# Bucketed attention and two MLPs: queries and keys turned on the host, bits as plain float32 products on quarters of the array, values on halves of it in one long run for each three query tiles

## What is computed

```python
q_bits = (np.einsum('bhsd,dk->bhsk', q, proj) > 0).astype(np.int64)
k_bits = (np.einsum('bhsd,dk->bhsk', k, proj) > 0).astype(np.int64)
mask = q_bucket[:, :, :, None] == k_bucket[:, :, None, :]
scores = scale * np.matmul(q, k.transpose(0, 1, 3, 2))
scores = np.where(mask, scores, -1000000000.0)
scores = scores - np.max(scores, axis=-1, keepdims=True)
attn = np.exp(scores)
attn = attn / (np.sum(attn, axis=-1, keepdims=True) + 1e-09)
return np.matmul(attn, v).astype(np.float32)
```

## Time and profile before

| | us |
|---|---|
| median of 3 runs (817.24 to 818.34) | 817.36 |
| profiled execution, its own time | 818.54 |
| its span, first to last instruction | 816.8 |
| PE busy | 787.6 (96%) |
| DVE busy | 548.8 (67%) |
| ACT busy | 501.4 (61%) |
| POOL busy | 283.8 (35%) |

### The profile page before, as it was taken

One profiled execution on the slowest core, in us unless ns is written; L12 is line 12 of the kernel. 1 busy time (PEld: TensorE's weight loads), 2 busy tenths in 40 slices (PEclk: granted clock), 3 DMA queues, 4 the chain that ended last, 5 costly groups with the idle time before them and its releaser, 6 DMA issues.

```text
span 816.8 us, 13110 instructions
## 1 busy us (share of the span) xinstructions
PE 787.6 (96%) x3968; PEld 665.4 (81%) x3968; DVE 548.8 (67%) x929; ACT 501.4 (61%) x950; POOL 283.8 (35%) x457
## 2 busy tenths in 40 slices
PE   4999999999999889999999999999999999999998
PEld 4898888988888668888888888888888888888886
DVE  3899899989998678888988898893222322232223
ACT  2788887888889789877676688984222122212221
POOL 2887777877777844410000024442000000000000
PEclk9999999999999999999999999999999999999999
DMA  5221221222111233310000013331000100010001
GB/s 153 61 63 52 79 60 50 61 79 60 50 42 48 72 84 103 94 37 0 0 0 0 1 48 97 98 95 51 1 1 0 52 0 0 0 45 7 0 1 52
DMA packets 33568, 36.67 MB, mean 45 GB/s; under 512 B 3136, under 2 KB 25664, under 8 KB 33536
## 3 DMA queue, kind: packets, MB, share of 16 engines
q1 hardware_dynamic: 33536, 36.26, 15.7%
HBM read 26.22 MB, written 3.15 MB: 36 GB/s over the span
## 4 chain that ended last, share of the span: by engine, by line
PE 75%; DVE 8%; issue 7%; ACT 6%; POOL 2%; DMA 1%; ACTq 0%; DVEq 0%; SPq 0%; POOLq 0%
PE y_ps L954 32%; PE h_ps L888 10%; PE h_ps L889 10%; PE h_ps L887 10%; PE o_ps L866 4%; PE t_ps L854 3%; PE s_ps L844 2%; ACT probs L450 2%; ACT pt_hi L459 2%; DVE pt_lo L655 2%; PE s_ps L845 2%; DVE neg_max L641 2%; PE p_ps L817 1%; DVE q_main L635 1%; DVE o_pair L664 1%
## 5 line engine op out<-in xcount | busy, mean ns | idle before, releaser
L728 DVE SCALAR_TENSOR_TENSOR t_abs<-t_abs,h_ps 128x512 f32<-128x512 f32 x48 | 33.0, 688 | 187.1 <-ACT t_abs L525 187.1
L399 POOL TENSOR_TENSOR slot<-w_raw,slot 128x512 fp32r<-128x512 f32 x64 | 81.5, 1293 | 206.2 <-ACT slot L478 206.2
L525 ACT ACTIVATE t_abs<-h_ps,three_col 128x512 f32<-128x512 f32 x48 | 33.1, 689 | 191.1 <-PE h_ps L889 191.0
L887 PE MATMUL h_ps<-x_hi,slot 128*128 (+1 forms) x384 | 150.1, 391 | 0.2 <-DVE t_num L709 0.2
L889 PE MATMUL h_ps<-x_hi,slot 128*128 (+1 forms) x384 | 150.2, 391 | 0.0
L888 PE MATMUL h_ps<-x_lo,slot 128*128 (+1 forms) x384 | 150.0, 391 | 0.0
L954 PE MATMUL y_ps<-g_hi,slot 128*128 128x512 f32 x384 | 126.2, 390 | 0.4 <-DVE g_lo L734 0.4
L954 PE MATMUL y_ps<-slot,g_hi 128*128 128x512 f32 x384 | 118.3, 389 | 0.0
L450 ACT ACTIVATE probs<-s_ps,exp_bias,exp_scale 128x768 f32<-128x768 f32 x96 | 95.5, 995 | 35.4 <-POOL exp_bias L386 34.7
L655 DVE TENSOR_TENSOR pt_lo<-t_ps,pt_hi 128x384 fp32r<-128x384 f32 x192 | 97.3, 548 | 17.9 <-ACT pt_hi L459 16.8
L641 DVE TENSOR_REDUCE neg_max<-s_ps 128x1 f32<-128x768 f32 x96 | 91.5, 953 | 11.3 <-PE s_ps L845 10.0
(11 more groups left out here) (102 smaller groups left out, 1416.6 us busy)
## 6 DMA issues: line engine op xcount, KB each, us to landing
w_raw<-in_moe_w_in SPq DMA_DIRECT2D x32, 256.0 KB, 2.7
w_raw<-in_moe_w_out SPq DMA_DIRECT2D x32, 256.0 KB, 2.7
raw_qk<-in_q SPq DMA_DIRECT2D x16, 192.0 KB, 2.4
raw_qk<-in_k SPq DMA_DIRECT2D x16, 192.0 KB, 2.5
raw_v<-in_v SPq DMA_DIRECT2D x16, 192.0 KB, 2.4
q_main<-q_cross SPq DMA_DIRECT2D x16, 192.0 KB
k_main<-k_cross SPq DMA_DIRECT2D x16, 192.0 KB
out<-t_den SPq DMA_DIRECT2D x6, 256.0 KB, 2.1
```

What stands on the lines that cost most here:

```text
L399: nc.gpsimd.tensor_tensor(slots[f][:, j, 1, :], w_raw[j][:, :], slots[f][:, j, 0, :].bitcast(F32), ALU.subtract).then_inc(w_lo_made, 1)
L887: mm(h_ps[b][:, :], w_hi, x_hi[:, kt, cols], start=(kt == 0), stop=False)
```

## The change

The host hands over queries and keys as (batch, head, 64, 768), with the tokens in the order in which the kernel takes them. One head's queries (rows 0 to 63) and keys (rows 64 to 127) are one tile `raw`. ACT copies it as the high part into `q_main` (`split_hi`), POOL subtracts for the low part into `q_cross` (`split_lo`), and SP moves the halves to where the score products want them (`place_head`, four transfers, and `place_bits`, four). `project` takes `raw` and the unsplit `proj` as plain float32: four products a pair of 32 columns of weights each, on four different quarters of the array's columns. DVE makes all bits of a pair in one operation (`threshold`), which goes through a tile `bits`.

The probabilities are copied as plain float32, one half of each tile by ACT, the other by DVE (`take_turned`). `weigh` multiplies them with the unsplit values, 64 columns of weights for each head, head 0 on the left half of the array's columns, head 1 on the right half. The output is then already the two heads' rows of `x`, and ACT and DVE split it straight from PSUM, one group of three query tiles at a time (`upper_x`, `lower_x`). The work of pair i is done during pair i+1: twelve products behind each other at tiles 2 and 8, right behind the transposes of the step. The scale of the scores moves from the copy of the keys into `bias`, whose second operation now needs the result of the first. All pairs are written out, there is no loop in this stage. Five weight slots are split during pairs 2 to 6, the others during the first MLP steps.

```diff
-    def heads_view(x):
-        return x.rearrange("b h (p t) d -> (b h) p (t d)", p=P)
-
-    q_dram, k_dram, v_dram = heads_view(q), heads_view(k), heads_view(v)
+    q_dram, k_dram = (x.rearrange("b h d n -> (b h) d n") for x in (q, k))
+    v_dram = v.rearrange("b h (p t) d -> (b h) p (t d)", p=P)
...
+    WEIGH_AT = {2: (0, 1, 2, 3, 4, 5)}
+    PROJECT_AT = TILES + 2
+
+    LAST_WEIGH = {2: (0, (0, 1, 2, 3, 4, 5)), 8: (1, (0, 1, 2, 3, 4, 5))}
+    LAST_X = {6: 2 * PAIRS - 4, 11: 2 * PAIRS - 3}
+
+    EARLY_SLOTS = 5
+    EARLY_PAIR = PAIRS - 1 - EARLY_SLOTS
+    EARLY_AT = (4, 8)
...
+            def place_head(h):
+
+                u = h % 2
+                sp.wait_ge(hi_made, h + 1)
+                move(k_main[u][0:D, :], q_main[u][D:P, :]).then_inc(moved_in[u], 16)
+                move(k_cross[u][0:D, :], q_main[u][D:P, :]).then_inc(moved_in[u], 16)
+                if h > 0:
+                    sp.wait_ge(lo_made, h + 1)
+                    move(k_cross[u][D:P, :], q_cross[u][D:P, :]).then_inc(moved_in[u], 16)
+                    sp.wait_ge(moved_in[u], 48 * (h // 2 + 1) - (16 if u == 0 else 0))
+                move(q_cross[u][D:P, :], q_main[u][0:D, :]).then_inc(main_in[u], 16)
...
+            def place_bits(h):
+
+                i, u = divmod(h, 2)
+                sp.wait_ge(bits_made, i + 2 if h else 1)
+                for half in range(2):
+                    cols = slice(HALF * half, HALF * (half + 1))
+                    at = QUAD * (2 * u + half)
+                    move(q_main[u][D:KROWS, cols], bits[at:at + MASKROWS, :]).then_inc(main_in[u], 16)
+                    move(k_main[u][D:KROWS, cols], bits[at + MASKROWS:at + 2 * MASKROWS, :]).then_inc(main_in[u], 16)
...
-                nc.gpsimd.tensor_scalar(exp_scale[:, r:r + 1], neg, MATCHED, 1.0, ALU.is_lt, ALU.mult)
-                nc.gpsimd.tensor_scalar(exp_bias[:, r:r + 1], neg, MATCHED, neg, ALU.is_lt, ALU.mult)\
+                nc.gpsimd.tensor_scalar(exp_scale[:, r:r + 1], neg, MATCHED, SCALE, ALU.is_lt, ALU.mult)\
+                    .then_inc(matched, 1)
+                alone(matched, n + 1)
+                nc.gpsimd.tensor_scalar(exp_bias[:, r:r + 1], neg, exp_scale[:, r:r + 1], 1.0, ALU.mult, ALU.mult)\
                     .then_inc(biased, 1)
...
+                    if j % TILES == 1 and h + 1 < NHEAD:
+                        split_lo(h + 1)
...
+            def split_hi(h):
+
+                i, u = divmod(h, 2)
+                act.wait_ge(raw_in[i % 2][u], 32 * (i // 2 + 1))
+                after(act, scored, TILES * (h - 1))
+                nc.scalar.activation(q_main[u][:, :], raw[i % 2][u][:, :], ACT.Copy).then_inc(hi_made, 1)
...
+                if t == 0 and 3 <= h < NHEAD - 1:
+                    upper_x(h - 3)
+                if n >= 1:
+                    exponentials(n - 1, j - 1)
+                if t == 0 and h + 1 < NHEAD:
+                    split_hi(h + 1)
+                if n >= TURN_LAG:
+                    take_turned(n - TURN_LAG)
...
+            def take_turned(n):
+
+                i, j = divmod(n, 2 * TILES)
+                u, t = divmod(j, TILES)
+                dve.wait_ge(turned, 2 * n + 2)
+                freed_by(dve, i, u, t // GROUP)
+                c = P * (t % GROUP)
+                nc.vector.tensor_copy(pt(i, u, t // GROUP)[:, GROUP:TILES, c:c + P],
+                                      t_ps[1][:, 0:HALF].rearrange("p (k q) -> p k q", k=GROUP))\
+                    .then_inc(pt_dve_made, 1)
...
+                for half in range(2):
+                    at = QUAD * (2 * u + half)
+                    last = mm(p_ps[at:at + QUAD, 0:HALF], proj_pair[:, :],
+                              raw[i % 2][u][:, HALF * half:HALF * (half + 1)], start=True, stop=True)
...
+                for kt in some:
+                    for u in range(2):
+                        last = mm(weigh_bank(e)[D * u:D * (u + 1), 0:HALF], v_nat[i % 2][u][:, kt, :],
+                                  pt(i, u, g)[:, kt, :], start=(kt == 0), stop=(kt == TILES - 1))
...
+                scores(h, i, u, n, j, t)
+                if n >= TURN_LAG:
+                    for half in range(2):
+                        turn_probs(n - TURN_LAG, half)
+                if i == PAIRS - 1 and j in LAST_WEIGH:
+                    weigh(i - 1, *LAST_WEIGH[j])
+                if 1 <= i < PAIRS - 1 and t in WEIGH_AT:
+                    weigh(i - 1, u, WEIGH_AT[t])
+                if j == PROJECT_AT and i + 1 < PAIRS:
+                    project(i + 1, 0)
+                    project(i + 1, 1)
...
+            pe.wait_ge(x_ready, 2 * PAIRS - 2)
+            hidden(0, 0, 0, 0)
+            for n in (NTILE - 3, NTILE - 2):
+                for half in range(2):
+                    turn_probs(n, half)
+            weigh(PAIRS - 1, 0, tuple(range(TILES)))
+            for half in range(2):
+                turn_probs(NTILE - 1, half)
+            hidden(1, 0, 0, 1)
+            weigh(PAIRS - 1, 1, tuple(range(TILES)))
```

More of the change, by code:

```diff
@@ L374, in _, with split_lo @@
-            pool.wait_ge(first_split, 4)
-            pool.sem_inc(qk_step, 4)
-            for part in range(4):
-                split_qk(1, 0, 1, part)
+            def split_lo(h):
+                u = h % 2
+                alone(hi_made, h + 1)
+                nc.gpsimd.tensor_tensor(q_cross[u][:, :], raw[h // 2 % 2][u][:, :], q_main[u][:, :].bitcast(F32),
+                                        ALU.subtract).then_inc(lo_made, 1)
             def bias(n, j):
@@ L510, in _ @@
-            with act.Fori(1, PAIRS - 1) as i:
-                for j in range(2 * TILES):
-                    step(i, j)
             def read_h(m, n, b):
@@ L630, in mask_rows @@
[L630 to L636 removed]
+            nc.vector.memset(proj_pair[:, :], 0.0).then_inc(proj_made, 1)
+            dve.wait_ge(proj_in, 32)
+            dve.wait_ge(proj_made, 1)
@@ new lines, in _, with threshold @@
+            nc.vector.tensor_tensor(k_cross[0][D:P, :], raw[0][0][D:P, :], q_main[0][D:P, :].bitcast(F32),
+                                    ALU.subtract).then_inc(lo_made, 1)
+            def threshold(i, rows=slice(0, P), first=False):
+                dve.wait_ge(bits_dot, 1 if first else i + 2)
+                if i >= 1:
+                    dve.wait_ge(main_in[1], 80 * i)
+                nc.vector.tensor_scalar(bits[rows, :], p_ps[rows, 0:HALF], bit_col[rows, 0:1], bit_col[rows, 1:2],
@@ L695, in _ @@
+            dve.wait_ge(bit_col_in, 32)
+            threshold(0, slice(0, D), first=True)
+            threshold(0, slice(D, P))
+            for i in range(PAIRS):
                 for j in range(2 * TILES):
@@ L903, in step @@
                 h, n = 2 * i + u, 2 * TILES * i + j
-                early, late = ((0, 1), (2, 3), (None, 4), (None, 5), (None, None), (None, None))[t]
-                ahead = within(h + 1, NHEAD)
-                if within(n, NTILE):
-                    scores(h, i, u, n, j, t)
-                if ahead and early is not None:
-                    prepare(h + 1, 1 - u, early)
-                if within(n - TURN_LAG, NTILE):
-                    for half in range(2):
-                        turn_probs(n - TURN_LAG, j - TURN_LAG, half)
@@ L914, in step @@
-                gj, third = divmod(j - WEIGH_LAG, GROUP)
-                if within(4 * i + gj, NGROUP):
-                    weigh(4 * i + gj, 2 * i + gj // 2, gj, third)
-                if ahead and late is not None:
-                    prepare(h + 1, 1 - u, late)
-            pe.wait_ge(dve_setup, 1)
-            pe.wait_ge(sel_made, 9)
-            for part in range(6):
-                prepare(0, 0, part)
-            for j in range(2 * TILES):
-                step(0, j)
-            with pe.Fori(1, PAIRS - 1) as i:
+                scores(h, i, u, n, j, t)
```

534 lines of the change are left out of this document (202 added, 332 removed).

## The result

The changed kernel takes 846.56 us (median of 4 runs, 842.82 to 847.06), the kernel before 817.71 us beside it (4 runs): ratio 1.034, 95% interval 1.033 to 1.036. It is 3.4% slower, and outside the range. The profiled execution took 847.06 us with a span of 844.9.

What follows compares the result with a forecast made beforehand. A ring of all engines through two score buffers was taken to pace attention. Start -0.5, pair 0 -2.9, looped pairs -0.5, last pair -1.8 and tail +2.9 summed to -2.8 us: 815 us, 0.3% faster, range 790 to 838.

Steps and rivals of the forecast that it cites:

- The long run: Twelve plain float32 value products between scores of tiles 2 and 3 (8 and 9): 4.0 us, other engines standing still.
- rival 3: Column halves take turns in the value products: a run is 7.9 us, `project` 2.6, total 891 us; chance 11%.
- rival 1: Plain float32 products go at the float32r price: a run is 2.1 us, total 792 us; chance 20%.
- The ring: Attention tiles: all engines take turns through two score buffers; a lap is 3.94 us for two tiles, 1.97 a tile.
- A looped pair: Pairs 1 to 6: first half 15.6 us plus second half 17.5 us, 33.1 against 33.18 before.
- `split_lo` "comes at tile 1 and is hidden behind the run at tile 2": POOL's 768-column subtraction in a looped pair: 2.0 us, fully hidden behind the run.
- "Four issues at 0.55 ... and 1.5 to land": Bit transfers after `threshold` bring operands 5.9 us after tile 9's maximum, wanted at 4.7; 0.6 us a pair added.
- rival 2: Placing of heads, SP's eight transfers each, becomes the bound: 822 us, or 838 with less overlap; chance 17%.
- The five early weights: Five early weight slots instead of six: costed at nothing; under one split, 3 us, if cover fails.
- Start: Time until tile 0: 14.9 us instead of 15.41, so -0.5 us.
- Tail: From tile 95 to `hidden(2)`: 21.3 us instead of 18.39, so +2.9 us.
- Theory B: Stated after the result: the run's standstill and lower clock set the pair; filling gaps at heads only exposes another wait.

Runs made afterwards that it cites:

- queue in order, bit products two tiles earlier: Changed kernel with loads ahead of head placing, second head's bits issued around the low move, bit products asked for after tile 6: 819.3 us, ratio 1.002.
- Halves apart: Kernel with queue in order and bit products two tiles earlier, each run issued as six left-half products then six right-half: 860.9 us, ratio 1.052.
- the run in pieces: Kernel with queue in order and bit products two tiles earlier, twelve value products cut into fours behind tiles 1, 2, 3: 806.9 us, ratio 0.986.
- earlier bit products: Bit products asked for one tile earlier in the changed kernel: 834.4 us; two tiles earlier in the kernel with queue in order: 819.3 us.
- the free bias: Kernel with the run in pieces, `exp_bias` computed without reading `exp_scale`: 803.4 us, ratio 0.981.
- finer pieces: Kernel with the free bias, products cut as four behind tile 1 and two behind each of tiles 2 to 5: 803.2 us, ratio 0.983.
- the loads first: Changed kernel with SP's loads (`v_nat`, early weights, `raw`) issued ahead of placing the second head: 832.8 us, ratio 1.019.

## Why the prediction failed, step by step

The step that failed is the placing of heads, which the sum put at nothing in the first half of a pair and at 0.6 us in the second; it cost 3.8 us a pair. Piece by piece the forecast comes close to the kernel in which placing is out of the way (queue in order, bit products two tiles earlier), in one piece partly by luck. In us:

| piece | forecast | changed kernel | placing out of the way |
|---|---|---|---|
| to tile 0 | 14.9 | 17.08 | 17.11 |
| pair 0 | 28.2 | 30.71 | 29.49 |
| looped pair | 33.1 | 36.87 | 33.07 |
| tile 84 to 95 | 29.3 | 30.70 | 29.21 |
| tile 95 to the end of the span | 543.0 | 545.18 | 543.65 |

(543.0 is 816.8 - 276.68 + 2.9.)

- **The long run, 4.0 us and 5.65 between maxima 2 and 3, 1.54 to the next**: right. 4.0, 5.59 and 1.40. (The 0.1 for changing the array's division stood on no row; between the run's last record and the scores 165.20 - 164.79 - 0.32 = 0.09 us go by.) Halves apart shows that the overlap is real, which rules out rival 3; rival 1 is out by the 0.32 us.
- **The ring, 3.94 us a lap with the wait for `exp_scale`**: the wait is 0.20 us on every tile, as said.
- **A looped pair, 15.6 + 17.5 against 33.07**: in pair 4 of the kernel with placing out of the way the halves take 15.58 and 17.36 us. The first is right, the second partly luck: it holds 0.6 for transfers that this kernel does not wait for, and nothing for the early weights. Pair 1, which has none of those, takes 30.97 us, pairs 2 to 6 take 33.49 on average. At the end of pair 4 there, POOL subtracts for a weight ahead of tile 10's scale, and the scores of the next head stand behind it:

```profile
173.29 1.29 POOL L405 TENSOR_TENSOR slot<-w_raw,slot 128x512 fp32r<-128x512 f32 x1
...
174.56 0.22 POOL L389 TENSOR_SCALAR exp_scale<-neg_max 128x1 f32<-128x1 f32 x1
...
176.50 0.47 PE L787 MATMUL s_ps<-k_cross,q_cross 128*128 128x512 f32 x1 [1.24 <-ACT probs L443]
```

  From the last maximum of the pair to the next is 2.86 us here and 1.59 in pair 1. No run leaves the early weights out, so their whole price stays open; with the run in pieces pair 1 is no shorter than the others (30.95 and 30.75).
- **`split_lo` "comes at tile 1 and is hidden behind the run at tile 2"** is the step that failed. Its 1.82 us on POOL are hidden; what follows on it is not. Two transfers in a row hang on it, with a landing between them, then four loads and four bit issues in SP's order: 9.85 us, of which the sum held nothing in the first half of a pair. Moving the loads out of it gave 14 us.
- **"Four issues at 0.55 ... and 1.5 to land"** was mis-sized. The 12-row issues take 0.71 to 0.80, 3.1 us in all; the landing is 1.3 to 1.6. The scores of pair 5 began 6.5 us after the maximum of tile 9, not 5.9. I had put the right number, 0.79, into rival 2 and priced it at 1.0 us a pair; earlier bit products gave 12 to 13 us for 7 turns of a pair, 1.8 each. I had not counted what a late head costs beyond its wait: the scores and transposes behind it at 1.2 GHz.
- **The five early weights "I cost at nothing"**: I looked at when slot 5 is needed, not at ACT waiting in order for `w_raw` inside attention: 9.3 us of waiting there, gone with the loads moved. How much of the 14 us was this and how much the bits' place, no edit splits; pair 1 without early weights gained 1.4 us in its first half and the others 2.3.
- **Start, -0.5**: +1.7. The four bit issues run from 10.84 to 14.05 and the first scores begin at 15.43; no experiment was made on it.
- **Tail, +2.9**: with `hidden(2)` at 24.65 us behind tile 95, not 21.3. `hidden(0)` and most of the next run go at the low clock after standstills, the run in 316.77 - 311.06 = 5.7 us instead of 4.0. To the end of the span it is +5.1.
- **Sum**: placing, with the loads in its queue, accounts for 846.6 - 819.3 = 27.3 of the 31.6 us by which the forecast was low; start, pair 0 and tail for the other 4.3. Rival 2 had the right mechanism and the right side, with 17%, but its 822 to 838 us were too low as well. "It decides from 1.6 us a pair": it cost 36.87 - 33.07 = 3.8, where I had counted one of the two heads and no clock.

Theory B is out as the cause of the 3.4%, but its one true part is large: the two runs of a pair cost 2.3 us more in one piece each than in three. The prediction took that standstill as given, and without it, once placing is out of the way, the change goes from no gain to 1.4% (1.9% with the free bias).

## What to carry to other kernels

When a change turns one operand transfer into a chain of them, write down the whole queue for each head: every issue at its own measured length, every landing that the next issue waits for, and every load that stands between, then ask who waits last, at each place where it occurs and not only at the busiest one. Loads that do not belong to the chain go ahead of it, not inside it; here that alone gave 14 us. Taking one wait away shows its worth only if the engine queued behind the next transfer is free: move the whole group before judging.

A long block of matmuls between two links of a ring costs its own time once and the engines' standstill again. Here three pieces instead of one run gave 12 us, and finer pieces nothing more that the medians show. And a little work placed on an engine of the ring (here the early weights on ACT and POOL) is not free because its result is needed late: it can stand in order ahead of a link of the ring.

## What the runs showed of the hardware

- A plain float32 product of 384 columns leaves two records 0.32 us apart, 0.64 us in all, and left and right column halves overlap fully if their products alternate (24 records in 4.0 us), but only for about 1.3 us where the program issues one half after the other (6.65 us).
- A transfer of 12 rows of 384 columns costs SP more to issue than one of 64 rows of 768: 0.71 to 0.81 us in the loop against 0.46 to 0.61. From the start of its issue to its landing the low move took 165.78 - 163.31 = 2.47 us. The Trainium skill (DMA: Bandwidth & Descriptors, Anatomy of one DMA — SWDGE (gpsimd) path) fits 2.0 us and the bytes over 436 GB/s for transfers that GpSimd issues, for 192 KB an estimate of 2.45. The trace agrees for this transfer, which SP issues; the median of `k_cross<-q_main`, of the same size, is 2.9.
- PE came back from waits of 1.84 and 2.26 us at 1.2 GHz in the changed kernel (behind the second, granted clock 0.50 from 173.14 to 175.69), while the same kind of wait (1.83 us) with the loads first was followed by scores at 2.4 GHz (1.00 from 183.57 to 184.40) and transposes that slowed (0.52 from 184.40 to 187.20). In the changed kernel the first 512-column score products of the two tiles behind the wait at 192.27 last 0.79 and 0.78 us; those at 196.97 last 0.50 again.
